# Attention with a two-layer feed-forward network on one core: part sums joined on VectorE, and an earlier way back for the row sums

## The reference

```
mask = q_bucket[:, :, :, None] == k_bucket[:, :, None, :]
scores = np.where(mask, scale * np.matmul(q, k.transpose(0, 1, 3, 2)), -1000000000.0)
attn = np.exp(scores - np.max(scores, axis=-1, keepdims=True))
attn = attn / (np.sum(attn, axis=-1, keepdims=True) + 1e-09)
x = np.matmul(attn, v)                     # 16 heads, then tokens x (heads * 64)
x = (max(x @ w_in1, 0) + alpha * min(x @ w_in1, 0)) @ w_out1
h = x @ w_in2;  out = (P(h) / (Q(h) + 1e-06)) @ w_out2
```

## Time and profile before

| | |
|---|---|
| median of three runs | 804.44 us |
| the profiled execution | 804.27 us, of which the span of the trace is 802.2 us |
| PE busy | 780.0 us, 97% of the span |
| DVE, ACT, POOL busy | 530.7, 357.7, 281.4 us |
| mean granted TensorE clock | 0.998 |
| turns (PE, L510) of heads 2 to 14 | 57.97, 72.77, 88.95, 103.75, 119.94, 134.73, 151.17, ..., 182.15, 196.95, 213.06, 228.33, 243.99 us |

### The profile page before, as it was taken

One profiled execution on the slowest core, in us unless ns is written; L12 is line 12 of the kernel. 1 busy time (PEld: TensorE's weight loads), 2 busy tenths in 40 slices (PEclk: granted clock), 3 DMA queues, 4 the chain that ended last, 5 costly groups with the idle time before them and its releaser, 6 DMA issues.

```text
span 802.2 us, 11727 instructions
## 1 busy us (share of the span) xinstructions
PE 780.0 (97%) x3820; PEld 583.7 (73%) x3820; DVE 530.7 (66%) x822; ACT 357.7 (45%) x588; POOL 281.4 (35%) x341
## 2 busy tenths in 40 slices
PE   8899999999998999999999999999999999999998
PEld 5456556565565678888888888887888888888886
DVE  6877667676772654345333533379888988888886
ACT  7344554554454310112111201157667666676673
POOL 7565664664864579400000077781000000000000
PEclk9999999999999999999999999999999999999999
DMA  4676675675582144100000033330000100000001
GB/s 126 166 185 162 159 186 138 156 195 130 149 206 47 54 150 119 41 1 0 1 1 14 0 92 92 100 94 3 1 1 1 53 1 1 1 18 35 1 1 52
DMA packets 34206, 58.85 MB, mean 73 GB/s; under 512 B 9900, under 2 KB 13780, under 8 KB 34164
## 3 DMA queue, kind: packets, MB, share of 16 engines
q1 hardware_dynamic: 31796, 53.15, 24.6%
q10 hardware_dynamic: 2368, 5.15, 2.6%
HBM read 29.59 MB, written 3.24 MB: 41 GB/s over the span
## 4 chain that ended last, share of the span: by engine, by line
PE 76%; DVE 6%; POOL 5%; issue 5%; DMA 4%; SPq 3%; ACT 1%; POOLq 0%; DVEq 0%; ACTq 0%
PE ps_h L1316 32%; PE acc L1348 32%; DMA work<-rden_scratch 3%; PE ps_o L584 3%; PE ps_a L499 2%; PE ps_s L554 2%; PE ps_s L559 2%; DVE row_max L1015 1%; DVE p_sum L1048 1%; PE ps_o L605 1%; POOL v_three L932 1%; POOL x_lo L946 1%; POOL lo L855 1%; PE ps_a L495 1%; DMA den<-den_scratch 1%
## 5 line engine op out<-in xcount | busy, mean ns | idle before, releaser
L1381 ACT ACTIVATE g_hi<-num 128x512 fp32r<-128x512 f32 x96 | 60.0, 625 | 207.6 <-PE acc L1348 203.3
L1451 DVE TENSOR_TENSOR g_lo<-num,g_hi 128x512 fp32r<-128x512 f32 x96 | 72.3, 753 | 78.7 <-ACT g_hi L1381 78.1
L726 ACT ACTIVATE p<-ps_s 128x768 f32<-128x768 f32 x96 | 77.6, 811 | 83.9 <-PE ps_s L559 61.4
L1015 DVE TENSOR_REDUCE row_max<-ps_a 128x1 f32<-128x384 f32 x180 | 92.0, 553 | 31.6 <-PE ps_a L499 29.0
L1316 PE MATMUL ps_h<-x_hi,w_late_in_hi 128*128 128x512 f32 x288 | 78.9, 394 | 0.0
L1316 PE MATMUL ps_h<-x_hi,w_late_in_lo 128*128 128x512 f32 x288 | 78.8, 394 | 0.0
L1316 PE MATMUL ps_h<-x_lo,w_late_in_hi 128*128 128x512 f32 x288 | 78.8, 394 | 0.0
L584 PE MATMUL ps_o<-p,v_use 128*64 128x384 f32 x384 | 74.5, 507 | 0.0
L1459 DVE TENSOR_SCALAR num<-ps_h,alpha_sb 128x512 f32<-128x512 f32 x48 | 36.0, 750 | 54.4 <-PE ps_h L1316 52.6
L1389 ACT ACTIVATE den_q<-ps_h,abs_b 128x512 f32<-128x512 f32 x48 | 33.0, 688 | 83.7 <-PE ps_h L1316 77.5
L1048 DVE TENSOR_TENSOR p_sum<-p 128x768 f32<-128x768 f32 x48 | 54.2, 1133 | 14.8 <-PE ps_o L605 9.9
(11 more groups left out here) (166 smaller groups left out, 1557.6 us busy)
## 6 DMA issues: line engine op xcount, KB each, us to landing
stage<-in_w_in SPq DMA_DIRECT2D x26, 256.0 KB, 2.7
stage<-in_w_out SPq DMA_DIRECT2D x26, 256.0 KB, 2.8
raw<-in_qk SPq DMA_DIRECT2D x15, 384.0 KB, 3.9
q<-hi SPq DMA_DIRECT2D x30, 192.0 KB
k<-hi SPq DMA_DIRECT2D x30, 192.0 KB
v_raw<-in_v SPq DMA_DIRECT2D x16, 192.0 KB, 3.8
work<-rden_scratch SPq DMA_DIRECT2D x16, 192.0 KB, 3.5
out<-y SPq DMA_DIRECT2D x12, 256.0 KB, 2.5
```

The lines of the kernel that those rows point to most:

```text
L726: nc.scalar.activation(halves(p[c][:]), ps_s[c % 2][:, :, 0:HALF], ACT.Exp, scale=float(D) ** -0.5).then_inc(s_exp, 1)
L1015: dve.tensor_reduce(row_max[slot][:, i, c:c + 1], ps_a[:, i, 0:HALF], AX.X, ALU.max).then_inc(s_a_free, 1)
L1381: nc.scalar.activation(g_hi[f % 2][:], num[f % 4][:], ACT.Copy).then_inc(s_ghi, 1)
L1451: dve.tensor_tensor(g_lo[f % 2][:], num[f % 4][:], g_hi[f % 2][:], ALU.subtract).then_inc(s_glo, 1)
```

## The change

Four edits are made, all in attention.

1. A new step `join` on DVE: behind `add(1)` it adds `p_sum[1]` onto `p_sum[0]` (128x768, both inputs and the output in SBUF). PE's `sums` then takes two part sums instead of three, 8 products instead of 12. The counters of `s_add` change with it (`ADDS` = 4 for a head instead of 3).
2. SP's order: in a pair, the statistics go first, then `store_sums`, the loads of the next raw data and values, and right behind them `turn_sums`, which before stood behind `fill_a_pen`. `reciprocals` on DVE moves from the end of `begin` = 4 to the end of `begin` = 2.
3. The table of a-chunks: a2 moves from the third step to the fourth, so that PE issues it behind the scores of chunk 5 instead of ahead of them. ACT issues its two transfers of `fill_a_hi` behind the exponential of chunk 5 instead of ahead of it. `x_high` is written one step earlier, with nothing between the two places.
4. Head 0: the first two chunks of scores of head 1 are made behind the products with the values of chunks 4 and 5.

```
@@ uses_of
-                        ([("a", 2, 2)] if more else [], [("a", 2, 3)] if more else []),
-                        ([], []),
+                        ([], [("a", 2, 3)] if more else []),
+                        ([("a", 2, 2)] if more else [], []),
@@ attention_sync, pair
-                        if left > 1:
+                        if first and u == 0:
                             load_raw(u, j + 2)
-                        if left:
                             load_v(u, j + 1)
+                        if left or u == 0:
+                            fill_stats(1 - u, j + u)
                         if not (first and u == 0):
                             store_sums(sp, 1 - u, j - 1 + u, h - 1, den_row[1 - u][:])
-                        if left or u == 0:
-                            fill_stats(1 - u, j + u)
+                        if left > 1 and not (first and u == 0):
+                            load_raw(u, j + 2)
+                        if left and not (first and u == 0):
+                            load_v(u, j + 1)
+                        if u == 0 and not first:
+                            turn_sums(sp, j - 1)
                         if left > 1 or (left == 1 and u == 0):
                             fill_a_pen(1 - u, h + 3)
                         if left == 1:
                             stage_early(2 + u)
-                        if u == 0 and not first:
-                            turn_sums(sp, j - 1)
@@ attention_tensor
-                    for n in range(KC // 2):
+                    for n in (0, 2):
...
-                                elif not (final and u == 1):
+                                elif not (first or (final and u == 1)):
...
+                                if first and c + 2 >= KC:
+
+                                    scores(1, 0, c + 2 - KC, c + 2)
@@ attention_scalar
-                            if c == 4 and u == 1 and not first:
-                                x_high(act, j - 1)
...
+                            if c == (4 if first and u == 0 else 3) and (left > 1 or (left == 1 and u == 0)):
                                 fill_a_hi(1 - u, h + 3)
                             if c == 3 and not last:
                                 copy_v(1 - u, j + u)
+                            if c == 3 and u == 1 and not first:
+                                x_high(act, j - 1)
@@ attention_vector
+                def join(h):
+
+                    dve.wait_ge(s_add, ADDS * h + 2)
+                    dve.tensor_tensor(p_sum[0][:], p_sum[0][:], p_sum[1][:], ALU.add).then_inc(s_add, 1)
...
+                                    if begin + group == 4:
+                                        join(h)
-                            if begin == 4 and u == 0 and not first:
+                            if begin == 2 and u == 0 and not first:
                                 reciprocals(dve, j - 1)
```

More of the change, by code:

```diff
@@ L268, in build_program @@
             USES = KC + 2
+            ADDS = KC // 2 + 1
             def uses_of(left, u, first_head, second_head):
@@ L597, in sums @@
                 def sums(h):
-                    pe.wait_ge(s_add, KC // 2 * (h + 1))
+                    pe.wait_ge(s_add, ADDS * (h + 1))
                     if due(h):
                         pe.wait_ge(s_sums, h)
-                    for n in range(KC // 2):
+                    for n in (0, 2):
                         for i in range(4):
@@ L605, in sums @@
                             m = pe.matmul(ps_o[rows, 1, 0:QUARTER], ones[:], p_sum[n][:, i * QUARTER:(i + 1) * QUARTER],
-                                          start=(n == 0), stop=(n == KC // 2 - 1))
+                                          start=(n == 0), stop=(n == 2))
                     m.then_inc(s_summed, 1)
@@ L723, in exponential @@
                     if due(h):
-                        act.wait_ge(s_add, KC // 2 * (h - 1) + c // 2 + 1)
+                        act.wait_ge(s_add, ADDS * (h - 1) + (1, 2, ADDS)[c // 2])
                         act.wait_ge(s_pv, KC * (h - 1) + c + 1)
```

## The result

The changed kernel takes 846.09 us (median of 4 runs, 844.02 to 850.46); the kernel before took 804.16 us beside it (4 runs). The ratio is 1.0529, with a 95% interval of 1.0481 to 1.0578: 42 us slower, and 17 us above the range. The profiled execution is the slowest of the four, 850.46 us with a span of 848.3. The direction was right and the size far off.

A forecast was written before the change was run, and what follows sets the result against it. First heads were taken as bound by the a3 reduces, second by POOL's chain from x_low. Terms 7.7 + 1.4 + 1.0 + 2.6 - 4.5 = +8.2, clock +6.8, on 804.4 gave 819 us, range 806 to 829.

The forecast's parts named there:

- turn = start of the a3 reduces + 6.0: In first heads, the a3 reduces set the turn: 8.80 + 6.0 = 14.8 us.
- First heads: Heads 2, 4, 6, 8, 10: lo delays the second add and join, a3 reduces 1.54 us later; five heads, +7.7 us.
- Second heads: Heads 3, 5, 7, 9, 11: a3 reduces at 10.48, turn at 16.48 instead of 16.19; five heads, +1.4 us.
- the one that waits gets the next turn: DVE's 128x768 add and POOL's SBUF instructions exclude each other, first come first served; the waiting one goes next.
- The clock: Heads 2 to 12: PE idles 2.5 us in each; five of eleven gaps halve the clock, 1.35 us each, +6.8 us.
- my own upper bound of 15: Clock term if all eleven gaps of heads 2 to 12 made the clock fall: +15 us.
- rival E: The clock falls in nearly each head, time above 829 us; chance 0.05.
- Heads 0 and 1: Join behind adds already waiting for POOL costs +1.3 us each; moving head 1's first scores costs and saves nothing.
- Head 12: lo already ahead of the add; the join puts the a3 reduces 1.3 later, less 0.3: +1.0 us.
- The end: Head 13 and behind: earlier turn -1.9, values' products without clock fall -1.6, fewer products with ones -1.0; together -4.5 us.
- The exclusive port: A 128x768 DVE add and a POOL instruction on SBUF exclude each other; reduces out of PSUM are unaffected.
- the 0.14 us at the end: At SBUF handovers the waiting side gets in 0.14 us before the other's end; otherwise some +4 us, 823.

The follow-up runs named there:

- run 4: The changed kernel with 12 unused products put into PE's idle gap ahead of a4 to keep it busy: 827.40 us, ratio 1.0298.
- run 11: The kernel before with only SP's new order and early reciprocals, plus lo in second heads waiting for the end of POOL's own normalise: 797.86 us, ratio 0.9912.
- run 12: The changed kernel, with lo in second heads waiting for the end of POOL's own normalise: 836.34 us, ratio 1.0413.
- run 6: The changed kernel with one added wait, POOL waiting for the join ahead of lo: 804.88 us, ratio 1.0013.
- run 10: The changed kernel with POOL waiting for the join ahead of lo, and head 1's first scores back in head 0: 803.98 us, ratio 0.9999.
- run 1: The kernel before with the join alone (8 products with ones instead of 12): 813.34 us, ratio 1.0116.
- run 7: The kernel before with only a2 moved behind the last scores: 807.03 us, ratio 1.0047.
- run 8: The kernel before with only SP's new order and the reciprocals in the second step: 800.05 us, ratio 0.9961.
- run 5: The changed kernel with a2 back at its old place, ahead of the last scores: 827.93 us, ratio 1.0308.
- run 2: The changed kernel without the join (12 products with ones), all other edits kept: 813.98 us, ratio 1.0122.

## Why the prediction was right, and where it failed

**The rule "turn = start of the a3 reduces + 6.0"** held with the clock at 1.00: 10.56 to 16.56 and 12.18 to 18.16 in run 4.

**First heads**: the chain came as written. The a3 reduces were forecast at 10.34 and came at 10.51, since PE's scores of chunk 4 came only 0.04 us earlier (4.00 us behind the turn of head 4) and not 0.31, and lo with them at 6.67 and not at 6.41; run 4 puts the turn without falls at 16.56, where I had 16.34. The term was +1.54 a head and is +1.75.

**Second heads, the step that failed first**: "the one that waits gets the next turn", read off two places where the next POOL instruction was v_three. With lo right behind normalise the add was passed over in all five second heads, and with lo kept back in runs 11 and 12 it wasn't. I had the add work from 7.0 and the join from 9.49, with x_low behind it. By the ends of their records less 0.96 us, the add worked from 8.75 and the join from 11.22, with x_low ahead of it, and the a3 reduces came at 12.11. My term was +0.3 a head; without the clock it is 18.16 - 16.19 = +2.0, so 8.4 us were missing over five heads. The trace of the kernel before had the counterexample. In head 1 the add came while pen ran, lo followed pen at once and kept its usual 1.82 us, and the add ended 0.82 us behind lo:

```profile
49.34 2.80 DVE L1048 TENSOR_TENSOR p_sum<-p 128x768 f32<-128x768 f32 x1
```

```profile
48.08 1.46 POOL L864 TENSOR_TENSOR pen<-bit,cst 24x768 fp32r<-24x768 f32 x1
49.51 1.82 POOL L855 TENSOR_TENSOR lo<-raw,hi 128x768 fp32r<-128x768 f32 x1
```

I had read one pair in detail and taken the others to repeat it; a look at every add that takes over 1 us would have found this one.

**The clock, the other step**: "not every such gap need do it. I take five of eleven". From head 1 on PE had thirteen gaps of 1.4 us and more, and behind each the clock fell; those of first heads were 2.1 us long, those of second heads 3.7, where I had 2.5 for both. I had forecast +6.8. Heads 2 to 12 lost 39.6 us by the turns, of which run 4's heads account for 5 x 1.75 + 5 x 1.97 + 0.9 = 19.5; the other 20 are the clock's (run 4's own heads, one of them with a fall, took 18.9 us less). That is above my own upper bound of 15, since a fall in a second head cost 2.2 us (20.34 - 18.16), not 1.35. This was rival E, at 0.05.

**Heads 0 and 1**: "costs and saves nothing that I can see" was wrong. The scores of head 1 were work that stood in a wait of PE; with them gone PE idled 2.30 us and most of head 0 ran at half the clock (0.53 from 34 to 45 us). Forecast +2.6 in all, measured +8.4. Heads 0 and 1 take 32.3 us together in run 6 and 27.9 in run 10, so by these two profiles 4.5 us are the move's; the medians of the two don't bear that size out.

**Head 12**: forecast +1.0 and measured +0.9 where the clock stayed up (run 4), +2.4 with a fall.

**The end**: forecast -4.5, measured 0.6 - 2.4 = -1.8. In head 13 the join met x_low and took 2.61 us, so the turn of head 14 came no earlier, while the later stretch did gain.

The misses in the order above, by the profiled spans: first heads 1.1, second heads 8.4, clock of heads 2 to 12 13.3, heads 0 and 1 5.8, head 12 nothing, end 2.7. That is 31 us, between the forecast +15 and the +46 of the profiled run (+42 by the medians). The direction was right for the reason given; that the time was 27 us above the forecast comes from these steps, the clock's the largest.

The exclusive port itself stands as predicted, and the rule of the Trainium skill (SBUF — State Buffer, "Who interferes with whom") agrees with it, but for the 0.14 us at the end: in all runs the waiting add or join ends 0.80 to 0.82 us behind the other's record, and it takes 0.96 us alone.

## What to carry to other kernels

An instruction on DVE with two SBUF inputs that fits an idle stretch by its length may not fit by its neighbours: look at what POOL does in that stretch, and give the late one the first turn with a wait (lo behind the join: 846 to 805 us with no work removed). Before you write down who goes next, look through the whole trace for the longest instances of the instruction, not at one period of it. Where a wait on PE grows, count what it does to the clock as well, and don't move away the products that filled it. Edits that alone cost 9 us, cost 3.5 and gain 3.5 can cost 42 together, so measure them one by one: here the early sums alone gained 0.4%, and with one wait 0.8 to 0.9%.

## What was not expected of the hardware

A waiting add is passed over when POOL's next instruction follows back to back, but not always. Behind a normalise that lo followed at once, the add (in run 1 the join) got in each time that it came up to 0.76 us behind the start of normalise (seven cases in runs 1, 7 and 8), and was passed over each time that it came 0.77 us or more behind it (29 cases, to 1.49 us). Behind pen, with lo next, it was passed over in all five cases, the kernel before among them, at 0.97 to 1.35 us. Behind x_low, with v_three next, an add or a join always got in, at up to 1.57 us. Behind lo, with v_three next, one got in 58 times, at up to 0.98 us, and an add was once passed over at 0.34 us (run 1, head 1), so 0.76 is no general figure. Nor does it decide whether lo's input is there first: in run 7 the hi that lo reads was done 0.13 us before the add came and the add got in, in run 5 it was done 0.52 us after and the add was passed over. What gives the next turn stays open; a wait of lo on its own predecessor's semaphore, for 0.2 us of idling, settled it here (run 11).

PE's idle gaps of 0.7 us and more between 40 and 290 us, in all fourteen profiles, against the mean granted clock of the 3 us that I read behind each (fallen: under 0.95):

```
gap of PE            gaps   fallen
0.7 to 1.2 us         56      0
1.2 to 1.5 us         16      1
1.5 to 1.9 us         23     13
1.9 to 2.4 us         31     27
3.3 us and more       10     10
```

The gap's length alone does not decide between 1.5 and 2.4 us: one of 1.57 us (run 2) was followed by 0.55, one of 2.40 us (run 6) by 1.00.
